# Channel attention and gated FFN on one core: five chunks of the first score sum taken as three fp32r products, w_out loaded behind the rows

## What is computed

```python
B, N, C = 2, 6016, 256;  d_ff = 2048
qn = q / (norm(q, axis=1) + 1e-6);  kn = k / (norm(k, axis=1) + 1e-6)
s = kn.transpose(0, 2, 1) @ qn / tau          # per batch, 256 x 256
a = exp(s - s.max(-1)); a /= a.sum(-1) + 1e-9
x = (v @ a).reshape(B * N, C)
h = x @ w_in                                  # 12032 x 2048
out = (h * sigmoid(h)) @ w_out
```

## Time and profile before

| | |
|---|---|
| runs, us | 1080.83, 1080.01, 1080.93 (median 1080.83) |
| profiled execution, us | 1080.67 |
| its span, us | 1078.6 |
| TensorE busy | 1072.0 us, 99% |
| VectorE, ScalarE, GpSimd busy | 724.1, 622.9, 35.6 us |
| bytes read from HBM | 41.16 MB, of them some 31 MB in the first 81 us |

### The profile page before, as it was taken

One profiled execution on the slowest core, in us unless ns is written; L12 is line 12 of the kernel. 1 busy time (PEld: TensorE's weight loads), 2 busy tenths in 40 slices (PEclk: granted clock), 3 DMA queues, 4 the chain that ended last, 5 costly groups with the idle time before them and its releaser, 6 DMA issues.

```text
span 1078.6 us, 12988 instructions
## 1 busy us (share of the span) xinstructions
PE 1072.0 (99%) x4824; PEld 905.4 (84%) x4824; DVE 724.1 (67%) x942; ACT 622.9 (58%) x781; POOL 35.6 (3%) x24
## 2 busy tenths in 40 slices
PE   8999999999999999999999999999999999999998
PEld 7888888888888888888899888888888888888997
DVE  5777588567567566566688777567566566566665
ACT  6787665565555555555666565555555555555654
POOL 2460000000000000000000000000000000000000
PEclk9999999999999999999999999999999999999999
DMA  9990000200200200200200200200200200200100
GB/s 337 392 402 21 1 1 1 78 1 1 79 1 1 78 0 0 73 0 0 79 1 1 74 1 1 79 1 1 79 1 0 78 0 0 73 0 1 39 1 34
DMA packets 26140, 54.06 MB, mean 50 GB/s; under 512 B 2544, under 2 KB 7408, under 8 KB 26096
## 3 DMA queue, kind: packets, MB, share of 16 engines
q1 hardware_dynamic: 25520, 52.83, 13.4%
q10 hardware_dynamic: 576, 0.66, 0.2%
HBM read 41.16 MB, written 12.32 MB: 50 GB/s over the span
## 4 chain that ended last, share of the span: by engine, by line
PE 93%; DMA 3%; ACT 2%; DVE 1%; issue 1%; SPq 0%; ACTq 0%; DVEq 0%
PE ps_o L416 16%; PE ps_o L418 16%; PE ps_o L417 16%; PE ps_h L383 14%; PE ps_h L381 14%; PE ps_h L382 14%; DMA qk<-k_dram 2%; ACT ps_h L515 2%; PE ps_o L344 1%; DMA wp_raw<-k_dram 1%; DVE square_sum L699 0%; PE ps_o L375 0%; PE ps_o L374 0%; PE ps_o L373 0%; PE ps_h L373 0%
## 5 line engine op out<-in xcount | busy, mean ns | idle before, releaser
L383 PE MATMUL ps_h<-b_hi,a_lo_rest 128*128 128x512 f32 (+1 forms) x504 | 194.1, 385 | 0.0
L382 PE MATMUL ps_h<-b_lo,a_hi_rest 128*128 128x512 f32 (+1 forms) x504 | 194.1, 385 | 0.0
L381 PE MATMUL ps_h<-b_hi,a_hi_rest 128*128 128x512 f32 (+1 forms) x504 | 194.0, 385 | 0.0
L814 DVE TENSOR_TENSOR h_b<-ps_h,u 128x512 f32<-128x512 f32 x96 | 66.4, 692 | 166.8 <-PE ps_h L383 166.6
L795 DVE TENSOR_TENSOR u<-ps_h,u 128x512 f32<-128x512 f32 x96 | 66.4, 691 | 142.3 <-PE ps_h L383 91.1
L611 ACT ACTIVATE h_a<-ps_h 128x512 f32<-128x512 f32 x96 | 57.4, 597 | 162.2 <-PE ps_h L383 162.2
L416 PE MATMUL ps_o<-g_hi_b,wo_hi 128*128 128x512 f32 (+1 forms) x384 | 148.0, 385 | 0.0
L417 PE MATMUL ps_o<-g_lo_a,wo_hi 128*128 128x512 f32 (+1 forms) x384 | 147.9, 385 | 0.0
L418 PE MATMUL ps_o<-g_hi_b,wo_lo 128*128 128x512 f32 (+1 forms) x384 | 147.9, 385 | 0.0
L416 PE MATMUL ps_o<-g_hi_a,wo_hi 128*128 128x512 f32 (+1 forms) x384 | 147.9, 385 | 0.0
L417 PE MATMUL ps_o<-g_lo_b,wo_hi 128*128 128x512 f32 (+1 forms) x384 | 147.8, 385 | 0.0
(11 more groups left out here) (117 smaller groups left out, 1533.2 us busy)
## 6 DMA issues: line engine op xcount, KB each, us to landing
v_raw<-v_t_dram SPq DMA_DIRECT2D x40, 256.0 KB, 3.7
out_t_dram<-v_raw SPq DMA_DIRECT2D x20, 512.0 KB, 3.2
qk<-q_dram SPq DMA_DIRECT2D x15, 384.0 KB, 11.0
qk<-k_dram SPq DMA_DIRECT2D x15, 384.0 KB, 11.2
wp_raw<-q_dram SPq DMA_DIRECT2D x8, 384.0 KB, 11.1
wp_raw<-k_dram SPq DMA_DIRECT2D x8, 384.0 KB, 11.6
home<-q_dram SPq DMA_DIRECT2D x6, 384.0 KB, 10.8
home<-k_dram SPq DMA_DIRECT2D x6, 384.0 KB, 10.7
```

What stands on the lines that cost most here:

```text
L381: nc.tensor.matmul(ps_h[:, bank, 0:n], w_hi, x_hi, start=start, stop=False, skip_group_check=True)
L382: nc.tensor.matmul(ps_h[:, bank, 0:n], w_hi, x_lo, start=False, stop=False, skip_group_check=True)
L383: return nc.tensor.matmul(ps_h[:, bank, 0:n], w_lo, x_hi, start=False, stop=stop, skip_group_check=True)
```

## The change

Chunks 7, 9, 11, 13 and 15 of batch 0 (`SPLIT`) are no longer scored with fp32 matmuls. ScalarE rounds the chunk (128x1536) to fp32r into one of two new tiles `qk_parts`, GpSimd subtracts for the lo part, and TensorE takes for each row and half k_hi * [q_hi | q_lo] (512 columns) and k_lo * q_hi (256 columns), two chunks later than before: its order is 0 to 6, 8, 7, 10, 9, 12, 11, 14, 13, 16, 17, 15, 18 and so on. ps_s[0] now takes two banks with 512 columns each, and `scale_scores(0)` adds the halves first. A slot of a split chunk is free to be loaded again when GpSimd is through. The w_out quarters are loaded behind all 34 chunks, when GpSimd is through with the w_in quarter that lies there; VectorE rounds them, two behind `add_rows(1)` and two behind the second `find_max`, and GpSimd subtracts them last. `sum_norms(1)` moves from behind fold 0 to behind fold 1. ScalarE waits for chunk 15 to be scored before `round_v(0, 0)`, and for the four w_out differences before its first copy of a fold of batch 1.

```diff
+SPLIT = (7, 9, 11, 13, 15)
+LAG = 2
+SETS = 2
...
+    ORDER = sorted(range(len(CHUNKS)), key=lambda g: (g + LAG, 1) if g in SPLIT else (g, 0))
...
-        ps_s = [ps_o[:, 0, :], ps_o[:, 1, :]]
+        ps_s = [[ps_o[:, 0, :], ps_o[:, 3, :]], [ps_o[:, 1, 0:C], ps_o[:, 1, C:2 * C]]]
...
                 if g >= RING:
-                    sp.wait_ge(chunk_scored, g - RING + 1)
+                    if g - RING in SPLIT:
+                        sp.wait_ge(rows_split, SPLIT.index(g - RING) + 1)
+                    else:
+                        sp.wait_ge(chunk_scored, PLACE[g - RING] + 1)
...
-                if g in (7, 10, 13, 16):
-                    n = (g - 7) // 3
-                    sp.dma_start(w_raw[:, n, :].rearrange("p (f c) -> p f c", c=C), w_out_parts[n]).then_inc(
-                        wo_loaded[n], 16)
...
-                    sp.wait_ge(wo_split, n + 1)
                     sp.dma_start(w_raw[:, n, :], w_in_parts[n // 2, n % 2]).then_inc(w_in_loaded[n], 16)
+            for n in range(PARTS):
+                sp.wait_ge(w_in_split, n + 1)
+                sp.dma_start(w_raw[:, n, :].rearrange("p (f c) -> p f c", c=C), w_out_parts[n]).then_inc(
+                    wo_loaded[n], 16)
...
+            def split_rows(n):
+                pool.wait_ge(rows_rounded, n + 1)
+                parts = [qk_parts[n % SETS][:, i].rearrange("p i r c -> p (i r c)") for i in range(2)]
+                nc.gpsimd.tensor_tensor(parts[1], qk[SPLIT[n] % RING][:, :, :, :].rearrange("p i r c -> p (i r c)"),
+                                        parts[0].bitcast(F32), ALU.subtract).then_inc(rows_split, 1)
...
+            def score_parts(g):
+                n = SPLIT.index(g)
+                pe.wait_ge(rows_split, n + 1)
+                parts = qk_parts[n % SETS]
+                for r in range(ROWS):
+                    for c in range(CK):
+                        hi, lo = (parts[:, i, 1, r, c * P:(c + 1) * P] for i in range(2))
+                        nc.tensor.matmul(ps_s[0][c], hi, parts[:, :, 0, r, :], start=False, stop=False,
+                                         skip_group_check=True)
+                        mm = nc.tensor.matmul(ps_s[0][c][:, 0:C], lo, parts[:, 0, 0, r, :], start=False, stop=False,
+                                              skip_group_check=True)
+                mm.then_inc(chunk_scored, 1)
...
-                if group == 0:
+                if group == 1:
                     sum_norms(1)
...
+            def round_rows(g):
+                n = SPLIT.index(g)
+                if n >= SETS:
+                    act.wait_ge(chunk_scored, PLACE[SPLIT[n - SETS]] + 1)
+                nc.scalar.activation(qk_parts[n % SETS][:, 0], qk[g % RING][:, :, :, :], ACT.Copy).then_inc(rows_rounded, 1)
...
                     if opening and pair == 0:
+
+                        act.wait_ge(wo_split, PARTS)
                         for group in range(FOLDS // 2):
                             copy_folded(1, group)
...
                 square_chunk(g)
-                if g in (9, 12, 15, 18):
-                    round_wo((g - 9) // 3)
+                if g in SPLIT:
+                    round_rows(g)
                 if g == SECOND + 2:
+
+                    act.wait_ge(chunk_scored, PLACE[SPLIT[-1]] + 1)
                     round_v(0, 0)
...
+            def round_wo(n):
+                dve.wait_ge(wo_loaded[n], 16)
+                nc.vector.tensor_copy(wo_part(wo_hi, n), w_raw[:, n, :]).then_inc(wo_rounded, 1)
...
+                    if b == 0:
+                        link(nc.vector.tensor_copy(scores[:, c, :], ps_s[b][c][:, C:2 * C]))
+                        link(nc.vector.tensor_tensor(scores[:, c, :], total, scores[:, c, :], ALU.add))
+                        total = scores[:, c, :]
...
             add_rows(1)
+            for n in range(PARTS // 2):
+                round_wo(n)
             shift_norms(1)
             invert_q()
             scale_scores(1)
             find_max()
+            for n in range(PARTS // 2, PARTS):
+                round_wo(n)
             sum_a(0, 0)
             invert_sums(1)
             split_a(0, 0)
```

More of the change, by code:

```diff
@@ L55, in channel_attention_ffn @@
     SECOND = ENDS[0]
+    ORDER = sorted(range(len(CHUNKS)), key=lambda g: (g + LAG, 1) if g in SPLIT else (g, 0))
+    PLACE = [ORDER.index(g) for g in range(len(CHUNKS))]
+    assert all(CHUNKS[g][0] == 0 and CHUNKS[g][2] == ROWS and g + LAG < SECOND for g in SPLIT)
     WIDE = N // (2 * TOK)
@@ L100, in channel_attention_ffn @@
         t_raw = sb("t_raw", [P, 2, TOK])
+        with ExitStack() as early:
+            qk_parts = [sb(f"qk_parts{n}", [P, 2, 2, ROWS, C], F32R, stack=early) for n in range(SETS)]
         b_hi = [sb("b_hi0", [P, FACTORS, TOK], F32R)]
@@ L161, in channel_attention_ffn @@
         chunk_added = sem("chunk_added")
+        rows_rounded = sem("rows_rounded")
+        rows_split = sem("rows_split")
         rows_added = sem("rows_added")
@@ L306, in _ @@
             nc.gpsimd.memset(square_sum[1][:], 0.0).then_inc(sums_cleared, 1)
[L308 to L311, removed]
+            def split_rows(n):
[3 more added lines that the diff above has]
+                                        parts[0].bitcast(F32), ALU.subtract).then_inc(rows_split, 1)
+            for n in range(len(SPLIT)):
+                split_rows(n)
             pool.wait_ge(v_loaded, 64)
@@ L334, in _ @@
                                         ALU.subtract).then_inc(w_in_split, 1)
+            for n in range(PARTS):
+                pool.wait_ge(wo_rounded, n + 1)
+                nc.gpsimd.tensor_tensor(wo_part(wo_lo, n), w_raw[:, n, :], wo_part(wo_hi, n).bitcast(F32),
+                                        ALU.subtract).then_inc(wo_split, 1)
         @block.tensor
@@ L343, in score_chunk @@
                     for c in range(CK):
-                        mm = nc.tensor.matmul(ps_s[b][:, c * C:(c + 1) * C], qk[s][:, 1, r, c * P:(c + 1) * P],
-                                              qk[s][:, 0, r, :], start=(row + r == 0 and c == 0),
+                        mm = nc.tensor.matmul(ps_s[b][c][:, 0:C], qk[s][:, 1, r, c * P:(c + 1) * P], qk[s][:, 0, r, :],
+                                              start=(row + r == 0 and (b == 0 or c == 0)),
                                               stop=(row + r == R - 1), skip_group_check=True)
+                mm.then_inc(chunk_scored, 1)
[10 more added lines that the diff above has]
+                                              skip_group_check=True)
                 mm.then_inc(chunk_scored, 1)
@@ L472, in _ @@
                 nc.tensor.matmul(ps_turn[:, 0:P], ones[:], ones[:], start=True, stop=True)
-            for g in range(len(CHUNKS)):
-                score_chunk(g)
+            for g in ORDER:
+                if g in SPLIT:
+                    score_parts(g)
+                else:
+                    score_chunk(g)
                 if g == SECOND + 1:
@@ L551, in round_a @@
                 nc.scalar.activation(a_hi(pair)[:, 3:7, :], sums[:], ACT.Copy).then_inc(a_rounded, 1)
-            def round_wo(n):
-                act.wait_ge(wo_loaded[n], 16)
-                nc.scalar.activation(wo_part(wo_hi, n), w_raw[:, n, :], ACT.Copy).then_inc(wo_rounded, 1)
             def round_w_in(n):
@@ L721, in scale_scores @@
                 for c in range(CK):
-                    link(nc.vector.scalar_tensor_tensor(scores[:, c, :], ps_s[b][:, c * C:(c + 1) * C],
+                    total = ps_s[b][c][:, 0:C]
+                    if b == 0:
+                        link(nc.vector.tensor_copy(scores[:, c, :], ps_s[b][c][:, C:2 * C]))
+                        link(nc.vector.tensor_tensor(scores[:, c, :], total, scores[:, c, :], ALU.add))
+                        total = scores[:, c, :]
+                    link(nc.vector.scalar_tensor_tensor(scores[:, c, :], total,
                                                         k_scale[:, c:c + 1], q_scale[:], ALU.mult, ALU.mult))
```

## The result

The changed kernel takes 1090.14 us (median of 6 runs, 1089.66 to 1092.28) against 1080.62 for the kernel before in the same session: ratio 1.0091, 95% interval 1.0078 to 1.0104, so 9.5 us slower. The forecast was 1084.8, the range 1079.6 to 1087.3. The sign was right, the size less than half of what came.

The account below looks back on a forecast made before the run. TensorE bounds the kernel, busy 1072.0 of 1078.6 us. Products and squares 0, fold 7 later by 1.65, second pair of w_out differences 2.5: +4.1 us on 1080.67, or 1084.8; range 1079.6 to 1087.3.

Parts of the forecast that it names:

- the first pause: TensorE before the first split chunk's products: a stall of 1.8 us until GpSimd's difference is ready.
- The three later pauses of 0.1: TensorE before later split chunks: three more stalls of 0.1 us each, since ScalarE paces the pairs.
- the early differences: GpSimd's first two w_out differences, 89.6 to 94.3: q_scale of the batch 1 norms waits for them, +0.8 us.
- Part 3: w_out on VectorE and GpSimd: fold 7 1.65 us later, then 2.5 us more before TensorE's first product.
- the second pair: GpSimd's last two w_out differences, 99.9 to 104.6: they hold invert_sums(1), 2.5 us more.
- rival 1: VectorE's sum_a(0, 0) is held too: fold 7 +4.0 us for one difference, +6.4 for both; 1084.7 to 1087.1; chance 0.22.
- the main case: The second pair of w_out differences holds the two-column addition of invert_sums(1): +4.1 us, 1084.8; chance 0.35.
- the worst case: Both late w_out differences hold sum_a(0, 0) before fold 7: +6.4 us, 1087.1.
- Part 2: The chain of squares on ScalarE and VectorE: without w_out among the rows, row sums end at 88.3 instead of 90.94.

Follow-up runs that it names:

- no_late_diff: The changed kernel without the last two of GpSimd's four w_out differences (that half's lo part is zero): 1085.69 us, ratio 1.0048 to the kernel before.
- filled_18: The changed kernel with 18 needless fp32r matmuls behind turn_probs(1), in TensorE's pause before fold 7: 1088.20 us (two runs).
- sums_first: The changed kernel with one wait more: GpSimd begins its sums of v only when add_rows(0) is done: 1089.30 us (two runs).
- products_only: The changed kernel with its five split chunks, but w_out loaded, rounded and subtracted among the rows as before: 1084.07 us, ratio 1.0030 to the kernel before.
- all_fp32: The changed kernel with no split chunk, all chunks in fp32, no addition of halves, w_out still late: 1088.55 us, ratio 1.0063 to the kernel before.

## Why the prediction was wrong

Right, with its size: the products save 0.08 for each row and half (0.35 against 0.43), and the first pause takes most of it (I had 1.8, it was 1.53). For the end of chunk 18 I had 48.9 against 49.06, that is 0.2 gained; 0.45 came, of which 0.22 by the products. The three later pauses of 0.1 are not in the trace. Right in kind: roundings hidden behind the row sums, two on the path at 1.2 (I had 1.3), `sum_norms` one fold later at no cost, TensorE's gain eaten up by the early differences, the sign.

Wrong:

1. **Part 3, the second pair.** I let `sum_a(0, 0)` through and had only `invert_sums(1)` held, for 2.5 us, and put the other case into rival 1 with 0.22. Both first additions of `sum_a` were held, one for each difference, 4.2 us more, and by the time of `invert_sums(1)` (106.72) GpSimd was done. Rival 1 at its upper end, +6.4, is the mechanism; `no_late_diff` puts 4.5 us on it with its share of the clock. The rows before had no such operation beside GpSimd, and the main case put its hold at nothing all the same. The section of the Trainium skill that I had quoted beside it ("SBUF — State Buffer", "Who interferes with whom": a VectorE operation with two SBUF inputs contends with a GpSimd instruction that reads SBUF) holds: 2.44 and 2.31 against 0.28 and 0.29.
2. **The clock, assumed to stay.** I had taken a stretch of 3.80 us with 2.08 of work as the proof. A pause of 5.88 behind one of 2.14 is another matter. 1.9 us by `filled_18`, 2.25 by the distance from fold 7 to the first fold of batch 1. It had no place in any rival, and without it even rival 1's upper end (1087.1) falls short. With 5 us of idle time forecast for the worst case, the clock should have stood beside it.
3. **Part 2, the row sums at 88.3.** They ended at 90.48, 0.46 earlier than before instead of 2.6. I had left the two additions of `add_rows(0)` out of the chain, and they were held themselves by GpSimd's sums of v (0.85 and 1.64 for 0.69 each). ScalarE squared chunk 19 at 46.26, I had 44.2. `sums_first` gives back 1.0 us of it in the row sums and 0.8 in the time. By this GpSimd's early pair ended at 96.3 instead of 94.3, and the maximum at 100.38 instead of 98.65: 1.7 us, the rest of the gap. The pair itself took as long as forecast, 4.65 us from the end of the second rounding (91.69) to 96.34; but I had let q_scale wait for both differences, and it was through at the end of the first (94.08), while the two-column k_scale waited for the second.

From the forecast to the result: 2.3 for the second pair (6.4 against 4.1), 1.7 for the row sums and 2.2 for the clock, less 0.5 because the two held additions cost 4.2 and not the 4.7 of rival 1; that is 5.7, against 5.6 missing in the span.

## What to carry to other kernels

A helper engine that "has nothing to do" is not free: beside GpSimd's two-operand work on SBUF, price a VectorE addition of two SBUF tiles or an operation of a tile in SBUF with a scalar at up to the length of a whole GpSimd instruction, once for each that is queued, and put that work beside additions that read PSUM or beside a reciprocal. A stall that you forecast for TensorE can have a second price in its clock (in the profiled execution of `products_only` one of 2.30 us was enough). Where two chains end together, a saving on one is worth nothing before the work moved onto the other has been added up to the same point.

## What the runs showed that I had not expected

- A two-column operation (128x2, 0.17 us alone) waits as long as a wide one: 2.25 us.
- VectorE and GpSimd take turns on back-to-back work: with two differences queued, one operation of VectorE gets done at the end of the first (94.08, 103.93), and so two small operations pay for two differences. GpSimd's two differences take 5.17 and 5.07 us instead of 4.7, but not because of the held operations: in `all_fp32` the early pair takes as long with VectorE idle for 6.96 us behind its roundings. What lengthens the first one is the second rounding, which is still running when it starts (to 86.33 there).

```profile
85.81 5.08 POOL L359 TENSOR_TENSOR wo_lo<-wp_raw,wo_hi 128x1024 fp32r<-128x1024 f32 x2 [10.39 <-DVE wo_hi L764]
```

- VectorE's additions of squares, with one operand in PSUM, were not lengthened beside GpSimd: 1.82 us for two, with or without it.
- After 2.27 and 1.71 us of standing (`no_late_diff`) the clock was at 1.00 for the pauses themselves and 0.57 on average over the four microseconds of work behind them:

```profile
101.90:104.20 2.30, 0.66 (x4) 0.42 (x4) 2.20 (x9) 1.55 (x4) 0.00 (x0) 1.00 0.00 0
104.20:108.20 4.00, 3.93 (x10) 3.10 (x11) 1.89 (x6) 3.02 (x7) 0.00 (x0) 0.57 0.01 2
```
